# Attention with a norm and two gated MLPs on one Trainium2 core: row sums from pairs, an earlier inverse for the half heads, weight tiles further apart

## What is computed

```python
scores = q @ k.T / 8 + slope[h] * -(i - j)        # only 0 <= i - j < 128, else -1e9
scores = scores - max(scores, axis=-1)
attn   = exp(scores)
attn   = attn / (sum(attn, axis=-1) + 1e-9)
x      = heads side by side of attn @ v            # (4, 576, 512)
xn     = (x - mean) / sqrt(var + 1e-6) * g_ln
x      = x + relu(xn @ w_ch1) @ w_ch2              # 512 -> 2048 -> 512
h      = relu(x @ w_in)                            # 512 -> 1024
out    = (h * sigmoid(conv3(h, conv_w))) @ w_out   # 1024 -> 512
```

## Time and profile before

| | us |
|---|---|
| median of 3 runs | 806.03 (805.5 to 806.35) |
| the profiled execution | 807.84 |
| its span, first to last instruction | 806.0 |
| mean granted TensorE clock | 0.998 |

### The profile page before, as it was taken

One profiled execution on the slowest core, in us unless ns is written; L12 is line 12 of the kernel. 1 busy time (PEld: TensorE's weight loads), 2 busy tenths in 40 slices (PEclk: granted clock), 3 DMA queues, 4 the chain that ended last, 5 costly groups with the idle time before them and its releaser, 6 DMA issues.

```text
span 806.0 us, 17023 instructions
## 1 busy us (share of the span) xinstructions
PE 783.7 (97%) x5809; PEld 754.6 (94%) x5809; DVE 520.0 (65%) x1419; ACT 372.3 (46%) x1033; POOL 171.9 (21%) x165
## 2 busy tenths in 40 slices
PE   9989799999999999989999999999999999999998
PEld 5668789999999999989999999999998999999998
DVE  6785777873667776456777646213259888788862
ACT  6884465652346555224655522113244444444532
POOL 5677832210212121011212101111210111011100
PEclk9999999999999999999999999999999999999999
DMA  7653512211221230122123012303230202222001
GB/s 186 172 163 99 185 37 75 71 42 59 68 68 39 74 92 21 59 71 68 39 74 86 27 59 83 106 13 96 80 100 10 82 31 81 81 81 81 22 23 45
DMA packets 56494, 59.42 MB, mean 74 GB/s; under 512 B 25184, under 2 KB 43616, under 8 KB 55904
## 3 DMA queue, kind: packets, MB, share of 16 engines
q1 hardware_dynamic: 56416, 58.43, 24.5%
HBM read 44.25 MB, written 14.16 MB: 72 GB/s over the span
## 4 chain that ended last, share of the span: by engine, by line
PE 74%; issue 11%; DVE 8%; ACT 3%; POOL 3%; POOLq 0%; DVEq 0%; ACTq 0%
PE bank L1378 21%; PE bank L1380 20%; PE bank L1379 20%; PE bank L1317 3%; PE bank L1349 3%; PE bank L1331 3%; PE bank L1276 1%; PE bank L1302 1%; POOL small L684 1%; PE bank L1289 1%; DVE prob L1029 1%; ACT prob L805 1%; DVE small L1022 1%; DVE q_st L1116 1%; PE bank L1265 1%
## 5 line engine op out<-in xcount | busy, mean ns | idle before, releaser
L1378 PE MATMUL bank<-xn_hi,wa_hi 128*128 128x288 f32 x512 | 156.4, 306 | 2.7 <-issue 2.7
L1378 PE MATMUL bank<-h_hi,wb_hi 128*128 128x288 f32 x512 | 156.3, 305 | 1.1 <-DVE h_lo L1086 0.6
L1379 PE MATMUL bank<-xn_lo,wa_hi 128*128 128x288 f32 x512 | 152.1, 297 | 0.0
L1380 PE MATMUL bank<-xn_hi,wa_lo 128*128 128x288 f32 x512 | 151.8, 296 | 0.0
L1379 PE MATMUL bank<-h_lo,wb_hi 128*128 128x288 f32 x512 | 150.9, 295 | 0.0
L1380 PE MATMUL bank<-h_hi,wb_lo 128*128 128x288 f32 x512 | 150.7, 294 | 0.0
L835 ACT ACTIVATE h_hi<-bank 128x288 fp32r<-128x288 f32 x128 | 52.4, 409 | 173.1 <-PE bank L1380 172.2
L1086 DVE SCALAR_TENSOR_TENSOR h_lo<-bank,h_hi 128x288 fp32r<-128x288 f32 x128 | 58.2, 455 | 113.9 <-ACT h_hi L835 112.3
L1378 PEld LDWEIGHTS bank<-xn_hi,wa_hi 128*128 128x128 f32 x512 | 96.7, 189 | 4.2 <-issue 3.4
L1378 PEld LDWEIGHTS bank<-h_hi,wb_hi 128*128 128x128 f32 x512 | 96.5, 189 | 3.3 <-issue 2.0
L1379 PEld LDWEIGHTS bank<-xn_lo,wa_hi 128*128 128x128 f32 x512 | 96.9, 189 | 0.0
(11 more groups left out here) (132 smaller groups left out, 1679.0 us busy)
## 6 DMA issues: line engine op xcount, KB each, us to landing
k_raw<-qkT SPq DMA_DIRECT2D x48, 144.0 KB, 2.9
q_raw<-qkT SPq DMA_DIRECT2D x48, 144.0 KB, 2.9
x_in<-x_spill SPq DMA_DIRECT2D x8, 580.0 KB, 4.3
ch_in<-ch_spill SPq DMA_DIRECT2D x8, 580.0 KB, 5.2
x_spill<-xT SPq DMA_DIRECT2D x4, 1152.0 KB, 4.2
ch_spill<-ch_stage SPq DMA_DIRECT2D x32, 144.0 KB, 1.9
out<-out_stage SPq DMA_DIRECT2D x32, 144.0 KB, 1.8
wa_raw<-w SPq DMA_DIRECT2D x16, 256.0 KB, 3.7
```

The lines of the kernel that those rows point to most:

```text
L1378: nc.tensor.matmul(dst, w_h, a_h, start=start, stop=False)
L1379: nc.tensor.matmul(dst, w_h, a_l, start=False, stop=False)
L1380: last = nc.tensor.matmul(dst, w_l, a_h, start=False, stop=stop)
```

## The change

It has four parts.

1. The row sums of the exponentials go to the first element of a pair (sum, epsilon) for each row tile; POOL fills the second element with 1e-9 once, at the start, with one more memset and one more wait. In place of adding the constant 1e-9 to the sum, `half_inverse` and `normalise` add up the pairs with a `tensor_reduce` over the last axis. The inverse is then taken in place in `row_inv`.
2. `small` grows from 41 to 47 columns.
3. The delay of `half_inverse` on DVE falls from 1.78 to 1.4.
4. `W_PACE` rises from 1.0 to 1.5, so tiles 14 to 31 stand at groups 0.25, 1.75, ... 25.75 of "first" on ACT, POOL and SP (before: 0.25, 1.25, ... 17.25).

```diff
-W_PACE, W_AHEAD = 1.0, 6
+W_PACE, W_AHEAD = 1.5, 6
-        rows3 = small[:, 0:18].rearrange("p (i t) -> p i t", i=3)
-        row_min, row_sum, row_inv = (rows3[:, i, :] for i in range(3))
+        row_columns = small[:, 0:24]
+        row_min, row_inv = row_columns[:, 0:6], row_columns[:, 6:12]
+
+        sum_eps = row_columns[:, 12:24].rearrange("p (t i) -> p t i", i=2)
...
-            nc.gpsimd.memset(rows3[:], 1.0).then_inc(zeros_ready, 1)
+            nc.gpsimd.memset(row_columns[:], 1.0).then_inc(rows_clear, 1)
+            pool.wait_ge(rows_clear, 1)
+            nc.gpsimd.memset(sum_eps[:, :, 1], SUM_EPS).then_inc(zeros_ready, 1)
...
-                                         accum_out=row_sum[0:rows, t:t + 1]).then_inc(exp_ready, 1)
+                                         accum_out=sum_eps[0:rows, t, 0:1]).then_inc(exp_ready, 1)
...
                 dve.wait_ge(half_exp, tile_of_half(c, h, n - 1) + 1)
-                nc.vector.tensor_scalar_add(row_inv[:, r:r + n], row_sum[:, r:r + n], SUM_EPS).then_inc(half_sum, 1)
+                nc.vector.tensor_reduce(row_inv[:, r:r + n], sum_eps[:, r:r + n, :], AX, ALU.add).then_inc(half_sum, 1)
...
                 dve.wait_ge(exp_ready, NT * hd + t1)
-                nc.vector.tensor_scalar_add(row_sum[0:rows, t0:t1], row_sum[0:rows, t0:t1], SUM_EPS).then_inc(sum_step, 1)
+                nc.vector.tensor_reduce(row_inv[0:rows, t0:t1], sum_eps[0:rows, t0:t1, :], AX, ALU.add).then_inc(sum_step, 1)
                 dve.wait_ge(sum_step, step + 1)
-                nc.vector.reciprocal(row_inv[0:rows, t0:t1], row_sum[0:rows, t0:t1]).then_inc(sum_step, 1)
+                nc.vector.reciprocal(row_inv[0:rows, t0:t1], row_inv[0:rows, t0:t1]).then_inc(sum_step, 1)
...
-("HS", 0.3, "half_min"), ("HS", 1.78, "half_inverse"),
+("HS", 0.3, "half_min"), ("HS", 1.4, "half_inverse"),
```

More of the change, by code:

```diff
@@ L23 @@
 ACT = mybir.ActivationFunctionType
+AX = mybir.AxisListType.X
 P = 128
@@ L96 @@
 FIRST_HEAD_0, HEAD_SLOTS_0, LAST_NORM_0 = 8.5, 5.05, 56.2
-SMALL = 41
+SMALL = 47
 WARM_START = 7
@@ L333, in build @@
         small = sb("small", [P, SMALL], scope=one)
-        rows3 = small[:, 0:18].rearrange("p (i t) -> p i t", i=3)
-        row_min, row_sum, row_inv = (rows3[:, i, :] for i in range(3))
-        columns = small[:, 18:18 + DC + 1]
+        row_columns = small[:, 0:24]
+        row_min, row_inv = row_columns[:, 0:6], row_columns[:, 6:12]
+        sum_eps = row_columns[:, 12:24].rearrange("p (t i) -> p t i", i=2)
+        columns = small[:, 24:24 + DC + 1]
         g_col, minus_half = columns[:, 0:DC], columns[:, DC:DC + 1]
-        stats = small[:, 23:35].rearrange("p (i t) -> p i t", i=2)
-        mean_var = small[:, 35:39].rearrange("p (i t) -> p i t", i=2)
-        rstd = small[:, 39:41].rearrange("p (i t) -> p i t", i=2)
+        stats = small[:, 29:41].rearrange("p (i t) -> p i t", i=2)
+        mean_var = small[:, 41:45].rearrange("p (i t) -> p i t", i=2)
+        rstd = small[:, 45:47].rearrange("p (i t) -> p i t", i=2)
         ch_stage = sb("ch_stage", [P, DC, CH], scope=one)
@@ L385, in build @@
         w_loaded, w1_loaded = [sem(f"w_loaded{i}") for i in range(NSTAGE)], [sem(f"w1_loaded{n}") for n in range(NW1)]
-        w_hi_pool = sem("w_hi_pool")
+        w_hi_pool, rows_clear = sem("w_hi_pool"), sem("rows_clear")
         w_prep, w_hi_ready, w_split_dve, w_split_pool = sem("w_prep"), sem("w_hi_ready"), sem("w_split_dve"), sem("w_split_pool")
@@ L780, in half_exps @@
                     nc.scalar.activation(scores, scores, ACT.Exp, bias=row_min[0:rows, r:r + 1], scale=-1.0,
-                                         accum_out=row_sum[0:rows, r:r + 1]).then_inc(half_exp, 1)
+                                         accum_out=sum_eps[0:rows, r, 0:1]).then_inc(half_exp, 1)
             def half_pt_copy(c, h):
@@ L1122, in run @@
                           ("A", 0.1, "relu"), ("B", 0, "evac"), ("W", 0.8 if kind == "first" else 0.3, "w"),
-                          ("HP", 0.45 if kind == "prologue" else 0.3, "half_pt"), ("HS", 0.3, "half_min"), ("HS", 1.78, "half_inverse"), ("HO", 0.45 if kind == "prologue" else 0.3, "half_x")]
+                          ("HP", 0.45 if kind == "prologue" else 0.3, "half_pt"), ("HS", 0.3, "half_min"), ("HS", 1.4, "half_inverse"), ("HO", 0.45 if kind == "prologue" else 0.3, "half_x")]
                 ahead = batch + (kind in ("first", "steady"))
```

## The result

The changed kernel takes 799.05 us (median of 4 runs, 798.6 to 799.17) beside 805.85 us for the kernel before. The ratio is 0.9911, 95% interval 0.9900 to 0.9922: 0.9% faster, or 6.8 us. Forecast were 798.3 us and a range of 795.0 to 803.5.

A forecast was written before the change was run, and what follows sets the result against it. PE's own work was taken as the bound, with waits to win only before 130 us. Eight terms summed to -7.7 us: 807.84 profiled to 800.1, or 798.3 us for the median; range 795.0 to 803.5.

The forecast's parts named there:

- Term 1: Prologue: with the earlier inverse, PE's three waits on ch_stage of L796 go, -0.9 us.
- Term 2: Prologue at 48.5 us: PE's 1.9 us wait of L1302 shrinks as ACT's scaling is ready sooner, -1.0 us.
- term 3: Prologue at 60 us: PE's wait on half_prob goes because the inverse is done earlier, -0.8 us.
- Terms 3 and 4: term 3, plus the 1.8 us wait of L1370 for the norm's inverse cut by 1.5 through POOL's new order.
- Term 5: Head 0: with 3.2 us of held L1022 off DVE's path and gaps on POOL, PE's waits shrink, -3.1 us.
- R1: Rival: the hold by POOL moves on from the sum to L1029, a tensor-scalar too; 803.1 us, chance 0.14.
- Term 6: Head 0: without two PE idles within three microseconds, the fall of the clock goes too, -1.7 us.
- R3: Rival: the waits go, but the clock falls all the same; 800.0 us, chance 0.08.
- Term 7: Head 1: the 1.3 us wait of L1349 behind a held L1029 pair stays, POOL being as busy, 0.
- Term 8: Heads 2 and 3: weight work newly placed there collides with DVE, a loss of 1.3 us.
- R2: Rival: the reduce is held like the tensor-scalar; about 799.6 us, chance 0.08.
- R5: Rival: spread weights carry head 0's pattern to heads 2 and 3, head 0 keeping it; 812.0 us, chance 0.06.

The follow-up runs named there:

- e1_reduce_only: The kernel before with the pair sum (tensor_reduce) alone, inverse at 1.78 and tiles 1.0 apart: 803.12 us.
- e2_inverse_only: The kernel before with the earlier inverse alone (half_inverse delay 1.78 to 1.4): 808.40 us.
- e4_no_reduce: The kernel before with the earlier inverse and tiles 1.5 apart, the constant still added to the sum: 804.42 us.
- e5_no_pace: The changed kernel with W_PACE back to 1.0, keeping pair sum and earlier inverse: 802.34 us.
- e3_pace_only: The kernel before with W_PACE raised from 1.0 to 1.5 alone: 802.97 us.

## Why the prediction was right, and where it was not

**The bound.** Right. (The eight rows that it adds up to 10.3 us are 11 waits, not 8.) Every microsecond gained ahead of 130 us came out at the end.

**Terms 1 and 2** (-1.9) against 2.47 measured from warm-up to first A product. Term 1 held in the trace: no wait on ACT's scaling is left. Term 2 was oversized in itself: the wait behind `first_x_tok` went from 1.9 to 1.3, not to 0.9. But both are credited to the wrong edit. With the pair sum alone and the inverse in its old place (e1_reduce_only) 1.7 of the 2.5 us are there already, and the wait of term 3 is gone as well: once the sum is not held, the old place is early enough for most of ACT's scalings. The earlier inverse added the other 0.8. But the reason given for the early place, that it "adds no wait" and only releases ACT, held only because of the pair sum. With the held sum in it the same place costs 1.4 to 1.8 us by the medians (e2_inverse_only, e4_no_reduce). I had costed the two edits one by one and seen no interaction.

**Terms 3 and 4** (-2.3) against 2.14. The stretch gives 0.9 with the pair sum alone and 1.2 with the pace alone. The wait for the norm's inverse went from 1.8 to 0.56, a gain of 1.2 where 1.5 was taken.

**Term 5** (-3.1) against 2.82. The size is right and the step is wrong. It said that 3.2 us of L1022 leave DVE's path because the reduce is not held, with POOL's gaps as a second reason. The runs show the gaps to be nearly the whole reason: with the pair sum and a dense POOL the 3.4 us sit on the scaling (e5_no_pace), and with the constant sum and gaps the longest L1022 is 0.6 us (e3_pace_only), with 5.0 of the 5.1 us gained in head 0. So rival R1 described what the pair sum does in head 0; the pace kept it from coming true. The argument against R1, that L1029 was never held for more than 1.4 us, was no argument: no L1029 had stood where L1022 stood.

**Term 6** (-1.7). Right in this kernel: the mean clock is 1.0 in all four of its runs, and it was 0.998 or less in all 48 runs of the kernel before that were timed with the experiments. R3 is out with it. The condition given for it does not hold in general: two idles within three microseconds came before the fall in the kernel before and in e5_no_pace, but in e1_reduce_only a single wait of 1.8 us did, and a wait of that length at that place brought no fall in the kernel before. What sets the two apart is open. Nor is the clock safe with the waits of head 0 short: e3_pace_only, with nearly the same ones there, had a mean clock of 0.998 in three of its six runs. Terms 5 to 7 together were -4.8, and 5.07 was measured.

**Term 7** (0) against some 0.6, the 2.25 us up to O less the 1.7 of the clock. The wait on `xT`, ahead of O of head 0 while head 1 is being scored, fell from 1.33 to 0.29: the pair of L1029 at 106.98 us that POOL held in the kernel before (1.64 us) met a gap of POOL, and took 0.62. A new wait of 0.34 on the minima took some of it back. **Term 8** (+1.3) against +1.11 by the sixth mark: the price of the spread tiles is real, and was well bounded by head 1. The extra memset moved POOL's first steps by 0.17 us; no effect of it on PE can be seen within the spread of the first mark.

**By edit, not by term.** The terms give the pair sum -4.8 (5 and 6), the earlier inverse -2.7 (1 to 3) and the pace -0.2 (4 and 8). Measured alone, by the ratios times 806 us, they are -3.5, +1.5 and -3.9, which add up to -5.9 where the three together gave -7.2. The sum came out near because all three were made at once: what was credited to the sum in head 0 was brought by the pace, and what was credited to the inverse in the prologue mostly by the sum. That part of the agreement is luck.

**The conversion.** The sum was -7.7 against a profiled execution 1.8 us above its median, and I kept that distance. The execution of the changed kernel (799.17) sits on its median, so the two traces differ by 8.6 us and the medians by 6.8. What the profiled execution of before had on top of its median I can't name: its clock, 0.998, was not lower than in the others. The forecast for the median was 0.8 us too good, that for the profiled execution, 800.1, was 0.9 us too high. The range does not quite follow from its own parts either: the terms named for its lower end give 795.5, not 795.0, and those for the upper end of the forecast's own case 800.9, not 801.5.

R2, R4 and R5 are out: the reduce is not held, the gains reach the end, and heads 2 and 3 gave back 1.1 us, not 10.

## What to carry to other kernels

A short operation that takes several times its usual time beside a busy GpSimd is held, and changing it alone can move the hold to the next operation of a form that can be held. List all such forms on the path, then either give them forms that are not held or thin out what holds them; here the first was worth 5.5 us and the second 2.8 to 4, and behind the first only some 1.6 us were left for the second. And before a step is moved ahead of others on its queue, ask how long it can take at worst, not usually: the same move was worth 1.2 us or cost 1.8. Last, an edit of three parts that comes out at the forecast says little of each part until each has run alone.

## What the runs showed of the hardware

A held tensor-scalar does not always get in when the running GpSimd operation ends. In head 0 it waited through two boundaries of back-to-back operations, 3.38 us, and again 3.31 us for a pair in e5_no_pace. The 2.28 us of L982 in e4_no_reduce are a third case, past the ends of two POOL operations at 56.36 and 56.88 us. In other places it got in at the first. What decides it is open, and was not tried. The Trainium skill (SBUF — State Buffer, "Who interferes with whom") speaks of a wait for the whole instruction that holds the port; these waits were longer.
